# Twenty more unread matmuls in TensorE's program of a fused attention and mixture-of-experts kernel

## The chip, the cores and the metric

The kernel runs on one core of one Trainium2 chip. The metric is the device time of one execution in microseconds (us); lower is better. Five engines work side by side, each on its own instruction list, and meet through semaphores: TensorE (PE, with its weight loads shown as PEld), VectorE (DVE), ScalarE (ACT), GpSimd (POOL) and SyncE (SP, which issues most transfers here).

The chip grants TensorE's clock at one of two levels, 2.4 GHz or half of it, 1.2 GHz. The profile shows it as PEclk: 1.00 is 2.4 GHz, 0.50 is 1.2 GHz.

## The reference

Three stages feed each other: banded attention, a top-1 mixture of eight experts with a skip score, and a dense mixture of four experts.

```python
# attention: q, k, v are (2, 8, 768, 64)
scores = scale * np.matmul(q, k.transpose(0, 1, 3, 2))
scores = scores + bias[None, :, :, :]          # -slope * distance
scores = np.where(keep, scores, -1000000000.0)  # 8 global keys, 96 local ones
a = softmax(scores); attn_out = np.matmul(a, v)
x = attn_out.transpose(0, 2, 1, 3).reshape(B * S, H * D)   # 1536 x 512
# first mixture: rows with x @ w_skip > 0
e_idx = np.argmax(xc @ w_gate, axis=1)
y[mask] = gate_w[mask, None] * (np.maximum(xc[mask] @ w1[e], 0.0) @ w2[e])
out[do_compute] = xc + y
# second mixture: every row through all four experts
for e in range(E):
    out += p[:, e:e + 1] * (np.maximum(x @ w1[e], 0.0) @ w2[e])
```

## The kernel before

**Attention** works through 48 units `u`: eight groups `n` (two heads of one batch element) of six query tiles `i` each. For each unit TensorE does `scores` (L1841; each product three times, for the high and low parts of keys and queries), `probs_T` (transposes of the softmaxed tile, L1850) and `pv` (probabilities times values, L1865 and L1866). Between them stand `fill` (transposes of the next keys and queries, L1815), `outputs_T` (transposes of three finished output tiles, L1874) and `logits` (the gate's nine columns, L1884). VectorE masks and normalises; ScalarE takes exponentials and copies.

**The end of attention** is a chain that no other unit covers. VectorE's `normalise` (L1261 to L1268) makes the last three output tiles, TensorE transposes them (`outputs_T(NB - 1, 1)`), ScalarE copies the transposes to SBUF (L923), TensorE multiplies them with the gate weights (`logits(NB - 1, 1)`) and VectorE adds the result to the rest (L1289).

**The routing** follows. VectorE takes the argmax of the logits (L1422 to L1428). TensorE counts each token's rank in its expert (L1952 and L1955, thirteen small matmuls). VectorE makes twelve one-hot tiles of the ranks (L1438), TensorE turns them into lists of tokens (L1962, 24 matmuls of 8 columns) while they come, and GpSimd gathers the tokens of each expert from DRAM (L825). In the meantime TensorE collects the gate weights (L1971). The gathered rows are transposed (L2001), copied by ScalarE (L1010) and go through the experts.

**The first mixture** runs as blocks of twelve 512-column matmuls (L2032) on weight pieces that VectorE and ScalarE split into a high and a low part (L1174, L902). A piece's buffer is loaded again by SyncE once TensorE's block is done (L646). **The second mixture** is L2133 and L2154; it fills the time from about 250 us to the end, almost all on TensorE.

Each engine runs its list in the order in which the code is written; a waiting instruction holds back everything behind it on its engine. There is no planner.

`unread(n)` (L1793 to L1797) issues `n` matmuls of 512 columns in bf16, with `ones_b` as both operands. They write PSUM bank 3, and what they write is read by nobody. The kernel before calls it with 9 at the very start, with 3 and 7 behind the scores of units 0 and 1. Eight more of the same kind, written out at L1968 (five) and L1975 (three), write bank 7. Bank 3 also takes the transposed probabilities of odd units and later the rank counts.

`banded(pe)` waits until VectorE has computed a flag (L1201) and then reads it into a register; the branch `pe.If(f > 0)` follows it.

Of the kernel before, what the change touches and what calls it, by code (L numbers as in the profile page):

```python
# [25 lines left out]
P = 128  # L26
# [6 lines left out]
def build(nc, q, k, v, n_global, n_local, w_skip, w_gate, m1_w1, m1_w2, probs, m2_w1, m2_w2, out, t_d, xz_d):  # L33
# [4 lines left out]
    DM = H * D  # L38
    KD = DM // P
    E, _, F = m1_w1.shape  # L40
    KF = F // P
    E2 = m2_w1.shape[0]
# [18 lines left out]
    with ctx:  # L61
# [3 lines left out]
        def sb(name, shape, dt):  # L65
            return ctx.enter_context(nc.sbuf_tensor(name, shape, dt))
# [6 lines left out]
        ones_b = sb("ones_b", [P, P], BF16)  # L73
# [280 lines left out]
        ps = ctx.enter_context(nc.psum_tensor("ps", [P, 8, 512], F32))  # L354
# [175 lines left out]
        def banded(eng):  # L530

            eng.wait_ge(bias_ready, 1)
            return eng.value_load(flags[0:1, 0:1], min_val=0, max_val=1)

        def wait(eng, s, value):

            if not isinstance(value, int) or value > 0:
                eng.wait_ge(s, value)
# [39 lines left out]
        def group_bank(n, g):  # L578
            j = place[n, g]
            return 4 + j if j < 4 else 6 + j % 2  # L580
# [16 lines left out]
        def pt_count(u):  # L597

            return sum(by_act(w) == by_act(u) for w in range(u + 1))

        def pt_sem(u):
            return pt_act if by_act(u) else pt_dve
# [1187 lines left out]

        @block.tensor
        def _(pe):
            def unread(n):  # L1793

                for x in range(n):
                    pe.matmul(ps[:, 3, :].rearrange("p (a c) -> p a c", c=P), ones_b[:, :],  # L1796
                              ones_b[:, :].unsqueeze(1).broadcast_to([P, 4, P]), start=True, stop=True)  # L1797

            pe.wait_ge(const_p, 1)
            unread(9)  # L1800
            pe.wait_ge(const_p, 4)

            def bank_free(j):
                if j >= 4:
                    group_out(pe, j - 2)

            def transposed(n, g, src, loaded):
                c, bank = int(g[1]), group_bank(n, g)
                bank_free(place[n, g])
                if (n, c) == (0, 0):  # L1810
                    pe.wait_ge(ld_first["kq".index(g[0])], 32)
                else:
                    pe.wait_ge(loaded[n % 2], (n // 2) * 32 + 32)
                for x, t in enumerate(tiles(n, c)):
                    mm = pe.transpose(ps[:, bank, x * P:(x + 1) * P], src[n % 2][:, t, :], ident[:, :])  # L1815
                mm.then_inc(tr_done, 1)

            def fill(n, g):
                if g[0] == "k":
                    transposed(n, g, kn, ld_k)  # L1820
                else:
                    transposed(n, g, qn, ld_q)
# [30 lines left out]
            def pv(u):  # L1853
                n, i = u // NI, u % NI
                b, half = n % 2, i // 3
                if i == 0:
                    pe.wait_ge(ld_v[b], (n // 2) * 96 + 96)
                if i % 3 == 0 and n:
                    pe.wait_ge(o_done, 2 * n - 1 + half)
                pe.wait_ge(pt_sem(u), pt_count(u))  # L1860
                for h in range(2):
                    out_ = ps[:, 4 + half, (i % 3 * 2 + h) * VW:(i % 3 * 2 + h + 1) * VW]
                    if i:
                        prev = vn[b][:, 0, h, :] if i == 1 else vp[b][:, i - 2, h, :]
                        pe.matmul(out_, pt_sb[u % 3][:, 2 * h, :], prev, start=True, stop=False)  # L1865
                    mm = pe.matmul(out_, pt_sb[u % 3][:, 2 * h + 1, :], vn[b][:, i, h, :], start=(i == 0), stop=True)  # L1866
                mm.then_inc(pv_done, 1)

            def outputs_T(n, half):
                g = "xb" if half else "xa"  # L1870
                bank_free(place[n, g])
                pe.wait_ge(o_done, 2 * n + 1 + half)
                for x in range(3):
                    mm = pe.transpose(ps[:, group_bank(n, g), x * P:(x + 1) * P], xo[n % 2][:, 3 * half + x, :], ident[:, :])  # L1874
                mm.then_inc(tr_done, 1)

            def logits(n, half):
                pe.wait_ge(xo_cp, 2 * n + 1 + half)
                if not half and not n:
                    pe.wait_ge(ld_small, 48)  # L1880
                if not half:
                    wait(pe, lg_add, n)
                for t in range(3 * half, 3 * half + 3):
                    mm = pe.matmul(ps[:, 4, LG + t * (E + 1):LG + (t + 1) * (E + 1)], xoT[:, t, :], wg9[:, n // 2, :], start=True, stop=True)  # L1884
                mm.then_inc(lg_mm, 1)

            fill(0, "k0")
            fill(0, "q0")
            f = banded(pe)
            with pe.If(f > 0):  # L1890
                fill(0, "k1")
                fill(0, "q1")
                pe.wait_ge(v_ones, 4)
                for u in range(NU_):
                    n, i = u // NI, u % NI
                    scores(u)
                    if filled(u):
                        fill(*filled(u))
                    if u >= 1:
                        probs_T(u - 1)  # L1900
                    if n and i in (0, 3):
                        outputs_T(n - 1, i // 3)
                    if n and i in (1, 4):
                        logits(n - 1, i // 3)
                    if u >= 2:
                        pv(u - 2)
                    if u < 2:
                        unread((3, 7)[u])
                outputs_T(NB - 1, 0)
                probs_T(NU_ - 1)  # L1910
                pv(NU_ - 2)
                logits(NB - 1, 0)
                pv(NU_ - 1)
                outputs_T(NB - 1, 1)
                logits(NB - 1, 1)
            with pe.Else():
                pe.wait_ge(ld_small, 48)
                with pe.Fori(0, NI * B * H) as n:
                    pe.wait_ge(g_ld, n * 48 + 48)
                    pe.transpose(ps[:, 0, P:2 * P], ident[:, :], ident[:, :])  # L1920
                    pe.transpose(ps[0:D, 0, 0:P], g_q, ident[:, :])
                    for c in range(NI):
                        mm = pe.transpose(ps[0:D, 1 + c // 4, (c % 4) * P:(c % 4 + 1) * P], g_k[:, c, :], ident[:, :])
                    mm.then_inc(g_t, 1)
                    pe.wait_ge(g_c, n + 1)
                    pe.matmul(ps[:, 3, :], g_qT[0:D, :], g_kT[0:D, 0:512], start=True, stop=True)
                    pe.matmul(ps[:, 4, 0:S - 512], g_qT[0:D, :], g_kT[0:D, 512:S], start=True, stop=True).then_inc(g_sd, 1)
                    pe.wait_ge(g_ex, n + 1)
                    for c in range(NI):
                        mm = pe.transpose(ps[:, 5 + c // 4, (c % 4) * P:(c % 4 + 1) * P], g_p[:, c * P:(c + 1) * P], ident[:, :])  # L1930
                    mm.then_inc(g_pt, 1)
                    pe.wait_ge(g_pc, n + 1)
                    for c in range(NI):
                        mm = pe.matmul(ps[:, 7, 0:D], g_pT[:, c, :], g_v[:, c, :], start=(c == 0), stop=(c == NI - 1))
                    mm.then_inc(g_pv, 1)


                pe.wait_ge(gx_ready, 1)
                for t in range(NT + 1):
                    if t < NT:  # L1940
                        for c in range(KD):
                            mm = pe.transpose(ps[:, t % 2, c * P:(c + 1) * P], X[:, t, c * P:(c + 1) * P], ident[:, :])
                        mm.then_inc(rt_tr, 1)
                    if t >= 1:
                        pe.wait_ge(rt_cp, t)
                        for c in range(KD):
                            mm = pe.matmul(ps[:, 2, (t - 1) * (E + 1):t * (E + 1)], xT[(t - 1) % 2][:, c, :], wg9[:, c, :],
                                           start=(c == 0), stop=(c == KD - 1))
                mm.then_inc(lg_done, 1)
# [3 lines left out]
            for t in range(NT):  # L1953
                n = NT - t
                mm = pe.matmul(ps[:, 3, (t + 1) * E:(NT + 1) * E].rearrange("p (t e) -> p t e", e=E), ones_b[:, :],  # L1955
                               oh_b[:, t, :].unsqueeze(1).broadcast_to([P, n, E]), start=False, stop=(t == NT - 1))
            mm.then_inc(rk_done, 1)

            for t in range(NT):
                pe.wait_ge(one_done, t + 1)  # L1960
# [237 lines left out]
```

## Time and profile before

| | us |
|---|---|
| median of three runs | 760.8 |
| lowest and highest | 760.09, 762.6 |
| the profiled execution, its own time | 762.36 |
| its span, first to last instruction | 760.6 |
| TensorE busy | 738.0 (97%) |
| VectorE busy | 465.7 (61%) |
| ScalarE busy | 324.7 (43%) |
| mean granted clock of TensorE | 0.983 |

Times in the rows count from the start of the span. A row of the timeline gives start, duration, engine, line, operation, what it writes and reads, how often, and in brackets how long the engine was idle before it and what ended that. Matmul durations include the way through the array, so a few in a row take less than the sum of their single times; the start of the next group shows the pace. A row of the chain gives start, duration and what the end of the span goes back to at that time.

### The profile page before, as it was taken

Reading aid. Unit: us, or ns where it says so; the run is one execution under the profiler, and the core shown is the slowest. Engines: PE = TensorE matmul, PEld = TensorE weight load, DVE = VectorE, ACT = ScalarE, POOL = GpSimd, SP = SyncE. Lnnn points to the kernel's source line nnn. Section 1 sums busy time; section 2 is a strip of 40 time slices with the busy share of each in tenths; the row PEclk is TensorE's granted clock in tenths of the full one; section 3 lists DMA queues with packets and bytes.
Section 4 is the critical chain, followed back from the end, with each engine's and each line's share of the span. In section 5 each row is a group of like instructions: output and inputs, shape, how many; then the busy total and the mean of one; then the engine's idle time right before and its main releaser. Section 6 shows DMA issues by size and latency. Waiting matters only on the chain.

```text
span 760.6 us, 11208 instructions
## 1 busy us (share of the span) xinstructions
PE 738.0 (97%) x4155; PEld 651.0 (86%) x4156; DVE 465.7 (61%) x932; ACT 324.7 (43%) x585; POOL 77.1 (10%) x114
## 2 busy tenths in 40 slices
PE   8999998799999799999999999999999999999996
PEld 4898897577888789899898998988989989899895
DVE  5776765699998966752752654563375275265442
ACT  3665665488987643331340431432333134042130
POOL 3101000116427000000000000000000000000203
PEclk8999999699999999999999999999999999999999
DMA  9769951799967220110020030020011003000102
GB/s 155 169 154 279 254 172 35 248 389 383 341 234 119 43 84 0 56 56 1 1 111 1 1 111 1 1 78 32 0 55 55 0 0 110 0 0 0 56 28 83
DMA packets 85969, 74.11 MB, mean 97 GB/s; under 512 B 52642, under 2 KB 58788, under 8 KB 85924
## 3 DMA queue, kind: packets, MB, share of 16 engines
q1 hardware_dynamic: 81924, 64.97, 28.2%
q0 software_dynamic: 3456, 8.43, 4.4%
q8 instruction: 25, 0.41, 0.2%
q10 hardware_dynamic: 544, 0.13, 0.1%
q14 instruction: 20, 0.16, 0.1%
HBM read 67.19 MB, written 6.33 MB: 97 GB/s over the span
## 4 chain that ended last, share of the span: by engine, by line
PE 89%; DVE 6%; ACT 1%; DMA 1%; issue 1%; SPq 0%; POOLq 0%; POOL 0%; DVEq 0%
PE ps L2154 34%; PE ps L2133 30%; PE ps L2032 9%; PE ps L1841 3%; PE ps L1866 2%; PE ps L1865 2%; PE ps L1850 2%; DVE piece_lo L1174 2%; PE ps L1815 2%; PE ps L1884 1%; PE ps L1874 1%; PE ps L2007 1%; DVE X L1268 1%; DVE ql L1225 1%; PE ps L1796 1%
## 5 line engine op out<-in xcount | busy, mean ns | idle before, releaser
L2133 PE MATMUL ps<-xs,w1s 128*128 128x384 f32 x1344 | 238.9, 337 | 3.8 <-ACT shared L1088 2.7
L2133 PEld LDWEIGHTS ps<-xs,w1s 128*128 128x128 f32 x1344 | 235.0, 189 | 6.6 <-ACT shared L1088 3.2
L2154 PE MATMUL ps<-w2s,h_hi 128*128 128x512 f32 x768 | 237.2, 390 | 0.0
L2154 PEld LDWEIGHTS ps<-w2s,h_hi 128*128 128x128 f32 x768 | 143.8, 188 | 29.1
L2154 PE MATMUL ps<-w2s,h_lo 128*128 128x512 f32 x384 | 149.9, 390 | 0.0
L1723 DVE SCALAR_TENSOR_TENSOR X<-ps,prn,X 128x512 f32<-128x512 f32 x84 | 63.1, 751 | 121.7 <-PE ps L2154 121.3
L1088 ACT ACTIVATE shared<-ps 128x384 f32<-128x384 f32 x96 | 45.8, 488 | 185.0 <-PE ps L2133 185.0
L1692 DVE TENSOR_TENSOR shared<-ps,shared 128x384 f32<-128x384 f32 x96 | 52.3, 556 | 92.7 <-ACT shared L1088 69.5
L2154 PEld LDWEIGHTS ps<-w2s,h_lo 128*128 128x128 f32 x384 | 72.1, 188 | 15.0
L1091 ACT ACTIVATE h_hi<-shared 128x384 fp32r<-128x384 f32 x96 | 49.7, 525 | 36.0 <-DVE shared L1692 36.0
L890 POOL DMA_INDIRECT out<-X,dst_i x12 | 11.6, 966 | 495.1 <-DVE X L1723 495.1
L1174 DVE TENSOR_TENSOR piece_lo<-ring,piece_hi 128x1024 fp32r<-128x1024 f32 x48 | 56.4, 1219 | 2.9 <-ACT piece_hi L902 2.8
L1698 DVE SCALAR_TENSOR_TENSOR h_lo<-shared,h_hi 128x384 fp32r<-128x384 f32 x96 | 50.2, 551 | 2.4 <-ACT h_hi L1091 0.5
L1245 DVE CUSTOM_DVE_ANT_0 area<-ps,shared 128x256 f32<-128x256 f32 (+1 forms) x96 | 34.7, 399 | 27.6 <-PE ps L1841 26.5
L931 ACT ACTIVATE area<-area,shared 128x256 f32<-128x256 f32 (+1 forms) x96 | 41.6, 482 | 21.9 <-DVE shared L1245 21.9
L902 ACT ACTIVATE piece_hi<-ring 128x1024 fp32r<-128x1024 f32 x48 | 48.0, 1057 | 0.0
L997 ACT ACTIVATE w2s<-raw 128x1024 fp32r<-128x1024 f32 x16 | 16.1, 1052 | 70.4 <-PE ps L2154 70.4
L2032 PE MATMUL ps<-piece_hi,xT_r 128*128 128x512 f32 x128 | 35.8, 403 | 1.0 <-ACT xT_r L1010 0.8
L2032 PE MATMUL ps<-piece_hi,hT_r 128*128 128x512 f32 x128 | 35.3, 399 | 1.1 <-DVE hT_r L1523 1.0
L1866 PE MATMUL ps<-X,raw 128*128 128x65 f32 x192 | 35.4, 273 | 0.0
L1865 PE MATMUL ps<-X,raw 128*128 128x65 f32 x160 | 30.1, 270 | 0.0
L2032 PEld LDWEIGHTS ps<-piece_hi,hT_r 128*128 128x128 f32 x128 | 23.3, 188 | 6.9 <-DVE hT_r L1523 2.4
(192 smaller groups left out, 834.0 us busy)
## 6 DMA issues: line engine op xcount, KB each, us to landing
ring<-in_moe_w SPq DMA_DIRECT2D x24, 1024.0 KB, 10.0
raw<-in_moe_w SPq DMA_DIRECT2D x16, 1024.0 KB, 5.1
shared<-in_moe_w SPq DMA_DIRECT2D x8, 1024.0 KB, 9.6
X<-in_v SPq DMA_DIRECT2D x16, 192.0 KB, 2.9
ys_d<-X SPq DMA_DIRECT2D x8, 384.0 KB, 3.3
X<-in_k SPq DMA_DIRECT2D x14, 192.0 KB, 4.1
shared<-in_q SPq DMA_DIRECT2D x14, 192.0 KB, 4.2
X<-in_v SPq DMA_DIRECT2D x16, 96.0 KB, 2.9
```

Of the source, the lines that this page charges most:

```text
L902: act.activation(unit(piece_hi[b % NHI], x), unit(piece_raw[b % NR], x), ACT.Copy).then_inc(p_hi, 1)
L1088: act.activation(part[:, slot, f, :], ps[:, 3 * f + BANK[ITEMS[item][0]], 0:HT], ACT.Copy).then_inc(copied, 1)
L1091: act.activation(h_hi[:, c, second * HT:second * HT + HT], src, ACT.Relu).then_inc(hd_hi, 1)
L1174: dve.tensor_tensor(unit(piece_lo[b % NR], x), unit(piece_raw[b % NR], x), unit(piece_hi[b % NHI], x).bitcast(F32), ALU.subtract).then_inc ...
L1692: dve.tensor_tensor(part[:, slot, f, :], ps[:, 3 * f + BANK[ITEMS[item][0]], 0:HT], part[:, slot, f, :], ALU.add).then_inc(added, 1)
L1698: dve.scalar_tensor_tensor(h_lo[c][:, here], src, 0.0, h_hi[:, c, here].bitcast(F32), ALU.max, ALU.subtract).then_inc(hd_lo, 1)
L1723: dve.scalar_tensor_tensor(X[:, t, :], ps[:, 6 + k % 2, :], p_, X[:, t, :], ALU.mult, ALU.add).then_inc(acc_done, 1)
L1865: pe.matmul(out_, pt_sb[u % 3][:, 2 * h, :], prev, start=True, stop=False)
L1866: mm = pe.matmul(out_, pt_sb[u % 3][:, 2 * h + 1, :], vn[b][:, i, h, :], start=(i == 0), stop=True)
L2032: mm = pe.matmul(ps[:, bank, :], src[xp][:, c0 + c, :], w[wp][:, c, :], start=(x == 0 and c == 0 and not (kind == "B" and half)), stop=(x ...
L2133: mm = pe.matmul(out_, w1s[:, wp, WI[name], c, f * P:(f + 1) * P], xs[:, 3 * b:3 * b + 3, xp, XI[name], c, :], start=(not onto and x == 0 ...
L2154: mm = pe.matmul(ps[:, 6 + k % 2, :], h_, w2s[:, wp, c, :], start=(x == 0 and c == 0), stop=(x == 2 and c == 3))
```

## The change

`unread` gets a second parameter, the PSUM bank, with 3 as its default. The first call issues ten instead of nine. Five calls are new: 2 between the first query transposes and the read of the flag, 3 ahead of the last `outputs_T`, 2 between it and the last `logits`, 9 behind these logits, and 3, on bank 7, behind the rank counts. That is 1 + 2 + 3 + 2 + 9 + 3 = 20 more matmuls. Nothing else moves.

```diff
         @block.tensor
         def _(pe):
-            def unread(n):
+            def unread(n, bank=3):
 
                 for x in range(n):
-                    pe.matmul(ps[:, 3, :].rearrange("p (a c) -> p a c", c=P), ones_b[:, :],
+                    pe.matmul(ps[:, bank, :].rearrange("p (a c) -> p a c", c=P), ones_b[:, :],
                               ones_b[:, :].unsqueeze(1).broadcast_to([P, 4, P]), start=True, stop=True)
 
             pe.wait_ge(const_p, 1)
-            unread(9)
+            unread(10)
             pe.wait_ge(const_p, 4)
...
             fill(0, "k0")
             fill(0, "q0")
+            unread(2)
             f = banded(pe)
             with pe.If(f > 0):
                 fill(0, "k1")
...
                 logits(NB - 1, 0)
                 pv(NU_ - 1)
+                unread(3)
                 outputs_T(NB - 1, 1)
+                unread(2)
                 logits(NB - 1, 1)
+                unread(9)
             with pe.Else():
...
             mm.then_inc(rk_done, 1)
+            unread(3, 7)
 
             for t in range(NT):
                 pe.wait_ge(one_done, t + 1)
```

TensorE's list at the start of the program, before and then after. `X` holds the first keys, `shared` the first queries; `TENSOR_LOAD flags` is the read of the flag.

```order
L1796 MATMUL ps<-ones_b 128x512 x9
L1815 MATMUL ps<-ident,X 128x128 x2
L1815 MATMUL ps<-ident,shared 128x128 x2
L533 TENSOR_LOAD flags
L533 ISA x2
L1890 COMPARE_AND_BRANCH
```

```order
L1796 MATMUL ps<-ones_b 128x512 x10
L1815 MATMUL ps<-ident,X 128x128 x2
L1815 MATMUL ps<-ident,shared 128x128 x2
L1796 MATMUL ps<-ones_b 128x512 x2
L533 TENSOR_LOAD flags
L533 ISA x2
```

One unread matmul more stands ahead of the first key transposes, and two stand between the first query transposes and the flag.

TensorE's list at the end of attention, before and then after. The rows of 65 columns are the last `pv`; L1874 is `outputs_T` and L1884 `logits`, three instructions each (the trace shows the three of `logits` as six). What follows the branch in the list is the other side of the `If`; on this input the engine goes on at the rank counts.

```order
L1865 MATMUL ps<-X,raw 128x65
L1866 MATMUL ps<-X,raw 128x65
L1874 MATMUL ps<-ident,X 128x128 x3
L1884 MATMUL ps<-wg,area 128x9 x3
L1890 UNCONDITIONAL_BRANCH
```

```order
L1865 MATMUL ps<-X,raw 128x65
L1866 MATMUL ps<-X,raw 128x65
L1796 MATMUL ps<-ones_b 128x512 x3
L1874 MATMUL ps<-ident,X 128x128 x3
L1796 MATMUL ps<-ones_b 128x512 x2
L1884 MATMUL ps<-wg,area 128x9 x3
L1796 MATMUL ps<-ones_b 128x512 x9
L1891 UNCONDITIONAL_BRANCH
```

Fourteen unread matmuls now stand around the last transposes and the last logits, nine of them ahead of the branch.

TensorE's list from the last rank counts to the gate weights, before and then after.

```order
L1955 MATMUL ps<-X,ones_b 128x16
L1955 MATMUL ps<-X,ones_b 128x8
L1962 MATMUL ps<-X 128x8 x24
L1968 MATMUL ps<-X,ones_b 128x512 x5
L1971 MATMUL ps<-X 128x24 x12
```

```order
L1959 MATMUL ps<-X,ones_b 128x16
L1959 MATMUL ps<-X,ones_b 128x8
L1796 MATMUL ps<-ones_b 128x512 x3
L1967 MATMUL ps<-X 128x8 x24
L1973 MATMUL ps<-X,ones_b 128x512 x5
L1976 MATMUL ps<-X 128x24 x12
```

Three unread matmuls now stand between the rank counts and the token lists; the five at L1968 stay where they were.

## Rows read from the trace of the kernel before

**Rows 1.** Stages: busy time of each engine (instructions), PEclk, DMA share, GB/s

```profile
0.00:20.00 20.00, 17.02 (x87) 9.82 (x89) 11.41 (x46) 7.88 (x17) 8.11 (x44) 0.83 0.93 147
...
130.00:147.00 17.00, 10.19 (x75) 6.35 (x76) 9.00 (x44) 7.05 (x9) 3.31 (x3) 0.60 0.58 184
...
265.00:760.60 495.60, 489.67 (x2471) 443.06 (x2469) 259.19 (x409) 148.60 (x272) 11.59 (x12) 1.00 0.10 36
```

**Rows 2.** Timeline of TensorE around the last outputs, the logits and the routing

```profile
126.91 0.52 PE L1874 MATMUL ps<-ident,X 128*128 128x128 f32 x3 [0.43 <-DVE X L1268]
...
131.44 0.87 PE L1874 MATMUL ps<-ident,X 128*128 128x128 f32 x3 [1.17 <-DVE X L1268]
132.89 1.45 PE L1884 MATMUL ps<-wg,area 128*128 128x9 f32 x6 [0.58 <-ACT area L923]
137.08 0.27 PE L1952 MATMUL ps<-X,upper_b 128*128 128x104 bf16 x1 [2.74 <-DVE X L1428]
...
138.82 2.00 PE L1962 MATMUL ps<-X 128*128 128x8 bf16 x24 [0.93 <-DVE X L1438]
141.06 1.91 PE L1968 MATMUL ps<-X,ones_b 128*128 128x512 bf16 x4 [0.24 <-issue]
```

**Rows 3.** The chain that ended last, from the last outputs to the first expert

```profile
122.99 0.57 PE ps L1884 x6
...
131.44 0.89 PE ps L1874 x3
...
132.89 1.46 PE ps L1884 x6
...
137.35 0.55 PE ps L1955 x12
...
138.82 2.02 PE ps L1962 x24
...
141.39 3.54 DMA area<-ys_d,tok_i
...
189.33 2.77 PE ps L2032 x12
```

**Rows 4.** Single microseconds, columns as in rows 1: where the granted clock changes

```profile
8.00:9.00 1.00, 0.88 (x5) 0.72 (x4) 0.87 (x3) 0.60 (x1) 0.38 (x2) 0.55 1.22 195
...
14.00:15.00 1.00, 1.00 (x4) 0.35 (x3) 0.88 (x2) 0.00 (x0) 0.80 (x2) 0.54 1.30 204
...
131.00:132.00 1.00, 0.56 (x3) 0.50 (x3) 0.29 (x1) 0.00 (x0) 0.00 (x0) 0.50 0.00 0
...
144.00:145.00 1.00, 0.94 (x4) 0.17 (x2) 0.00 (x1) 0.00 (x0) 0.06 (x1) 0.68 0.56 152
```

**Rows 5.** Timeline of TensorE in the first 16 us

```profile
1.07 3.88 PE L1796 MATMUL ps<-ones_b 128*128 128x512 bf16 x9 [1.07 <-POOL ones_b L756]
5.85 0.41 PE L1815 MATMUL ps<-ident,X 128*128 128x128 f32 x2 [0.90 <-DMA X<-in_k]
...
7.36 0.65 PE L1815 MATMUL ps<-ident,X 128*128 128x128 f32 x4 [0.89 <-DMA X<-in_k]
8.13 1.12 PE L1815 MATMUL ps<-ident,shared 128*128 128x128 f32 x4
...
12.83 2.72 PE L1796 MATMUL ps<-ones_b 128*128 128x512 bf16 x7
15.47 0.39 PE L1841 MATMUL ps<-kh,qh 64*128 64x256 f32 x2
```

**Rows 6.** Timeline of VectorE: two places at the start, and the one-hot tiles

```profile
10.25 0.29 DVE L1245 CUSTOM_DVE_ANT_0 area<-ps,shared 128x128 f32<-128x128 f32 x1 [0.79 <-PE ps L1841]
...
13.87 0.68 DVE L1225 SCALAR_TENSOR_TENSOR ql<-ps,qh 128x512 fp32r<-128x512 f32 x1
...
138.51 2.04 DVE L1438 TENSOR_SCALAR X<-iota_rb,area 128x128 bf16<-128x128 bf16 x12
```

**Rows 7.** Waits of SyncE's queue from 146 to 247 us

```profile
SPq L646 <- PE ps L2032: 48.1, 18, 3.3
```

## The prediction

> **What bounds the kernel now.** I read the stages first: from 265 us to the end TensorE is busy for 489.67 of 495.60 us at a granted clock of 1.00, and the change touches nothing there. Two stretches have a lower clock: the first 20 us (0.83) and 130 to 147 us (0.60), where TensorE is also idle for 6.8 of 17 us [rows 1]. The single microseconds show where the level changes: down at 8.1 us, up at 14.9, down at the start of 131, up in 144 [rows 4]. So 6.9 and 13.7 us run at 1.2 GHz. The chain of waits says what that costs: in 130 to 147 us it alternates between engines, and TensorE's pieces of it (transposes, logits, rank counts, token lists) have no cover [rows 3]. The timeline then gives the pauses into which the new matmuls go [rows 2, 5].
>
> The stages are coupled. An earlier expert stage starts its own transfers earlier, because SyncE loads a piece when TensorE has finished the block that held its buffer; SyncE's queue waits 48.1 us in all for that [rows 7]. Behind it TensorE is full. So I pass a gain ahead of 147 us on to the end at its full size, and a loss as well.
>
> **The price of one unread matmul.** At the low clock nine took 3.88 us, 0.431 each; 512 columns in that time are the 1.2 GHz level, although PEclk has no record of a change there yet [rows 5]. At the high clock no row shows an unread stream alone. The nearest is the expert blocks, twelve matmuls of 512 columns with their weight loads in 2.77 us, 0.231 each [rows 3]; I take it as the price.
> The Trainium skill (TensorE: Matmul & The Clock Gate, section "Wait — 56ns, not 53.3ns?") gives 426.7 ns and 215.7 ns start to start for 512 columns at the two levels. The first agrees with the 0.431 of rows 5; by the second the nine matmuls of the argmax would take an estimated 1.94 us instead of 2.08, and no step below would change sign.
>
> **The start: ten for nine, and two behind the first queries.** The tenth costs 0.23 to 0.43 us and lies in a pause of 0.90 us that ends with the landing of keys. The two cost 0.46 to 0.86 us and lie in the next pause, 0.89 us [rows 5]. Both are covered, by 0.03 us at worst. If the flag's read had to wait for the two, the four key transposes (0.65 us) could come late by some 0.3 us; the query transposes at 8.13 us wait for their own landing, so little of this reaches anyone. I take 0, bounds 0 and +0.3.
> Do they keep the clock from falling at 8.1? Between 5 and 8 us TensorE would still have pauses: of 1.79 us of idle time 0.7 to 1.3 are filled. I think the fall stays in most executions, and take 0 for it here as well; the other case is rival C.
>
> **The last outputs and logits.** In the trace the clock falls at 131.0, inside the 1.17 us for which TensorE waits for the last outputs, so everything behind it is at half speed [rows 2, 4].
> - The transposes take 0.87 us in the timeline; the same three, 0.52 at the high clock [rows 2]. Gain 0.35.
> - The logits take 1.46 us of the chain; the same six, 0.57 at the high clock [rows 3]. Gain 0.89.
> - Three unread ahead of the transposes: 0.69 us in a pause of 1.17, covered; at the low clock 1.29, so +0.12.
> - Two between them: 0.46 us in a pause of 0.58 (ScalarE's copy), covered with 0.12 to spare; at the low clock 0.86, so +0.28. ScalarE needs only the transposes' semaphore and isn't held up.
>
> **The nine during the argmax.** Ready for TensorE 2.74 us behind the logits are the one-hots that VectorE makes of them; that whole path is VectorE's, including a branch, and doesn't change its length. Nine take 2.08 us at the high clock: covered, with 0.66 us for TensorE's own branch behind them. At the low clock they take 3.88 us and the rank counts come 1.14 us late.
>
> **Rank counts and the three behind them.** The counts' chain pieces are 0.27 and 0.55 us [rows 2, 3]. No row has them at the high clock; their time falls between nothing and half, so 0 to 0.4, and I take 0.25, since both ratios above (0.52 to 0.87, 0.57 to 1.46) are large. Three unread behind them: 0.69 us in a pause of 0.93 in which VectorE turns ranks into one-hots; at the low clock 1.29, so +0.36. The 24 token-list matmuls take 2.02 us beside VectorE's twelve one-hots of 2.04 us [rows 3, 6]: VectorE sets that pace. 0 to 0.2, I take 0.1. The gather of 3.54 us behind them is a transfer [rows 3]: 0.
>
> **Sum.** If the clock is held from the last outputs through the rank counts: 0.35 + 0.89 + 0.25 + 0.10 = 1.59 us, with all 20 matmuls under cover. Against the profiled execution, 762.36 us, that is 760.8. The profiled execution is near the slowest of those known (760.09 to 762.6) and 1.56 above the median. Its clock fell almost as early as it could, 0.9 us behind the last attention matmul; an execution in which it falls later has less to win back. I give the median two thirds of the sum, 1.1 us: 760.8 - 1.1 = 759.7.
>
> **Rivals.**
> A, the forecast: held through the logits in most executions. 759.7, own range 759.0 to 760.5. For it: the longest pause of the stretch shrinks from 1.17 to 0.5 us, the pause of the argmax from 2.74 to 0.7.
> B, no measurable effect: 760.8, within 0.4. The clock may fall all the same between 130 and 137 us in about as many executions as before, since the transposes still wait for VectorE and ScalarE. Or it is held but falls at some 138 us, behind the rank counts, and is still low when the first expert starts: the row at 144 us shows it rising only just ahead of that [rows 4]. A low stretch of 3.4 us, half of the first one's 6.9, at 0.431 for 0.231 would cost 3.4 x 0.46 = 1.6 us, and take the gain back.
> The Trainium skill (same page, section "What's actually happening") describes the gate as free-running and not reset by a kernel's start, so that the moment of a change varies between runs. By that rule one trace can't promise the same 131.0 us for the next execution; the times of before, 2.5 us apart, agree with it, and it is why I cut the sum.
> C, the start is held too. Then the query transposes take 0.65 instead of 1.12 us and VectorE, idle for 0.79 us until the first scores, begins up to 0.75 us earlier; it is then busy until 14.55 (13.87 + 0.68) with what the third scores need, which begin at 15.47 only because seven unread at the low clock stand ahead of them (2.72 us; 1.6 at the high one). They could begin at 13.85: a gain of 1.6 us [rows 5, 6]. Time: 759.7 - 1.6 = 758.1. Against it: the pauses between 5 and 8 us are not filled.
> D, the other side: the clock is lost at 131 us as now and the nine are issued at 0.431. They leave cover at 2.74 / 9 = 0.304 us each, between both prices. Then the ranks are late by 1.14 us, and with the smaller overruns (0.12 + 0.28 + 0.36) by 1.90, and the routing, the gather and every expert with them. As the stream of nine may itself bring the clock back I take 1.5: 762.3.
>
> **How the numbers follow.** A 0.48, B 0.26, C 0.13, D 0.13. The likeliest is A: 759.7 us. About 0.3% (2.3 us) is what a measurement of this kernel can tell from no change: below 758.5 is faster, above 763.1 slower. C gives nearly all of faster, with the best executions of A: 0.18. D reaches 763.1 only in its worst form: 0.06. The rest, 0.76, is the same. The range from 758.0 to 762.3 takes in C's and D's values and leaves out their far ends.
>
> **What would show it.** PEclk at 1.00 from 131 to 137 us; the last transposes at about 0.5 us, the logits at 0.6; the pause ahead of the rank counts gone down to some 0.7 us, ended by VectorE still; the first expert 1.6 us earlier against the end of attention. If the rank counts follow the nine unread without a pause, D holds. If the clock is 0.50 at the first expert block, B's second form does. If the third scores begin near 14 us, C does. I am wrong altogether if the expert stage, started earlier, waits for weights: then TensorE would show idle time ended by transfers between 147 and 247 us, which it doesn't have now.

## The result and the profile after

The changed kernel takes 762.98 us (median of 20 executions, 759.47 to 764.28), the kernel before 761.53 in the same number (759.81 to 762.68). The ratio is 1.0018, with a 95% interval of 1.0009 to 1.0026: slower by 0.1 to 0.3%, outside the range that was predicted, where a gain of 1.1 us had been forecast. The profiled execution took 762.91 us, its span is 761.2.

The first 15 us went better than forecast. Timeline of TensorE of the changed kernel, same columns as [rows 5]:

```profile
5.80 0.61 PE L1815 MATMUL ps<-ident,X 128*128 128x128 f32 x2 [0.28 <-DMA X<-in_k]
...
6.47 0.59 PE L1796 MATMUL ps<-ones_b 128*128 128x512 bf16 x2
7.37 0.65 PE L1815 MATMUL ps<-ident,X 128*128 128x128 f32 x4 [0.31 <-issue]
8.10 0.66 PE L1815 MATMUL ps<-ident,shared 128*128 128x128 f32 x4
...
14.10 0.39 PE L1841 MATMUL ps<-kh,qh 64*128 64x256 f32 x2 [1.19 <-DVE ql L1225]
```

The keys' transposes start within 0.05 us of [rows 5]; the query transposes take 0.66 us instead of 1.12, and the third unit's scores start at 14.10 instead of 15.47, now 1.19 us after TensorE was ready for them. The clock isn't lost at 8 us.

The end of attention and the routing, answering to [rows 2]:

```profile
128.72 0.81 PE L1796 MATMUL ps<-ones_b 128*128 128x512 bf16 x3
130.05 0.52 PE L1874 MATMUL ps<-ident,X 128*128 128x128 f32 x3 [0.52 <-DVE X L1268]
130.40 0.59 PE L1796 MATMUL ps<-ones_b 128*128 128x512 bf16 x2
131.15 0.84 PE L1884 MATMUL ps<-wg,area 128*128 128x9 f32 x6
131.84 2.10 PE L1796 MATMUL ps<-ones_b 128*128 128x512 bf16 x9
134.73 0.22 PE L1956 MATMUL ps<-X,upper_b 128*128 128x104 bf16 x1 [0.79 <-DVE X L1428]
...
136.21 2.00 PE L1967 MATMUL ps<-X 128*128 128x8 bf16 x24 [0.26 <-DVE X L1438]
138.28 1.02 PE L1973 MATMUL ps<-X,ones_b 128*128 128x512 bf16 x4
140.67 0.49 PE L1976 MATMUL ps<-X 128*128 128x24 bf16 x12 [1.37 <-DVE X L1453]
141.01 1.44 PE L1980 MATMUL ps<-X,ones_b 128*128 128x512 bf16 x3
142.63 1.12 PE L2006 MATMUL ps<-ident,area 128*128 128x128 f32 x4 [0.18 <-DMA area<-ys_d,tok_i]
144.52 2.04 PE L2037 MATMUL ps<-piece_hi,xT_r 128*128 128x512 f32 x4 [0.78 <-ACT xT_r L1010]
146.37 1.91 PE L2037 MATMUL ps<-piece_lo,xT_r 128*128 128x512 f32 x4
```

All new matmuls are under cover: pauses of 0.52, 0.79 and 0.26 us are left, each ended by VectorE. But the first two groups of four 512-column matmuls of the first expert take 2.04 and 1.91 us, where before has 1.16 and 1.08. The stages tell why (columns as in [rows 1]):

```profile
130.00:144.00 14.00, 10.88 (x83) 5.57 (x84) 7.40 (x39) 6.67 (x9) 2.37 (x2) 0.83 0.71 221
144.00:148.00 4.00, 3.48 (x8) 2.81 (x9) 3.59 (x4) 0.38 (x1) 0.94 (x1) 0.50 0.92 312
148.00:152.00 4.00, 4.00 (x18) 3.20 (x17) 1.64 (x2) 0.87 (x2) 0.00 (x0) 0.80 1.01 386
```

The clock is at 2.4 GHz through the argmax and the rank counts, falls at 139.4 us, in the pause of 1.37 us ahead of the gate weights, and is at 1.2 GHz until 149.6 us, through the first five microseconds of the experts. The chain of waits gives each step its size. Of the changed kernel:

```profile
130.05 0.53 PE ps L1874 x3
...
131.15 0.85 PE ps L1884 x6
...
134.95 0.35 PE ps L1959 x12
...
136.21 2.01 PE ps L1967 x24
...
138.78 3.81 DMA area<-ys_d,tok_i
...
142.63 1.13 PE ps L2006 x4
...
144.52 6.73 PE ps L2037 x18
```

And of the kernel before, the two pieces of its chain that [rows 3] doesn't have:

```profile
144.98 0.68 PE ps L2001 x4
...
146.42 4.35 PE ps L2032 x18
```

| step | before | after | difference, us |
|---|---|---|---|
| last attention matmul ends (VectorE starts on it) | 130.29 | 128.89 | -1.40 |
| last transposes | 0.89 | 0.53 | -0.36 |
| last logits | 1.46 | 0.85 | -0.61 |
| rank counts | 0.82 | 0.57 | -0.25 |
| token lists | 2.02 | 2.01 | -0.01 |
| first gather, issue to landing | 3.54 | 3.81 | +0.27 |
| transposes of the gathered rows | 0.68 | 1.13 | +0.45 |
| 18 matmuls of the first expert | 4.35 | 6.73 | +2.38 |
| sum | | | +0.47 |

The transposes that follow start at 151.25 instead of 150.77: +0.48, so the table is complete to 0.01 us. 2.6 us are won ahead of the gather, and 3.1 given back in it and behind it.

The table compares two executions, and their spans differ by 0.6 us only (760.6 and 761.2), while the medians differ by 1.45. The profiled execution of before is one of its longer ones (its median span is 759.6), that of the changed kernel is close to its median (761.25). So some 0.9 us of the measured loss lies in the shorter executions of before, and of those there is no trace.

The 20 executions point the same way. Each one's span stands with its mean granted clock:

| kernel | mean clock: executions, spans in us |
|---|---|
| before (35 executions) | 0.990: 14, 758.1 to 759.1; 0.986: 13, 759.3 to 760.1; 0.988: 1, 761.2; 0.983: 7, 760.3 to 760.8 |
| changed (20 executions) | 0.997: 1, 757.7; 0.993: 5, 760.4 to 760.6; 0.991: 3, 759.5 to 761.5; 0.990: 3, 761.1 to 761.5; 0.988 and less: 8, 761.2 to 762.5 |

At 0.990, about 15 us recorded at the low level in both, the changed kernel's spans are 2.0 to 3.4 us longer. That points to what TensorE has to do while the clock is low, and not to how long it is low. The one execution in which it hardly fell is the fastest.

The mean clock needs care: the record has no entry before its first change and shows 1.00 until then. In the trace of the kernel with only the 17 matmuls from the last outputs on (below), TensorE's timeline has

```profile
7.36 1.11 PE L1815 MATMUL ps<-ident,X 128*128 128x128 f32 x4 [0.41 <-DMA X<-in_k]
...
14.97 0.38 PE L1841 MATMUL ps<-kh,qh 64*128 64x256 f32 x2
```

so these key transposes run at half speed (0.65 us in [rows 5]), and the seven unread matmuls at 12.9 us still take 2.14 us, where the changed kernel has 1.67 and before 2.72. The clock is low until about 14 us, an estimate from these three, and the record has no low entry there. The trace of before with 11 more shows the same. Low microseconds at the start can be missing from the mean clock of other executions too.

### The profile page after: what moved, and what is told of

It reads as the page before. It is cut to its first block, busy times and chain, and to the rows that moved or that the text cites. A ratio compares the mean times of both kernels' runs of the same rounds, so it can differ in the third digit from the quotient of the medians.

```text
span 761.2 us, 11248 instructions
## 1 busy us (share of the span) xinstructions
PE 741.0 (97%) x4175; PEld 651.9 (86%) x4176; DVE 465.7 (61%) x932; ACT 324.7 (43%) x585; POOL 77.2 (10%) x114
## 4 chain that ended last, share of the span: by engine, by line
PE 89%; DVE 7%; ACT 1%; DMA 1%; issue 1%; POOLq 0%; DVEq 0%; POOL 0%; SPq 0%
PE ps L2159 34%; PE ps L2138 30%; PE ps L2037 9%; PE ps L1841 3%; PE ps L1866 2%; PE ps L1865 2%; DVE piece_lo L1174 2%; PE ps L1850 2%; PE ps L1815 1%; PE ps L1884 1%; PE ps L1874 1%; PE ps L2012 1%; DVE ql L1225 1%; DVE X L1268 1%; DMA area<-ys_d,tok_i 1%
## 5 line engine op out<-in xcount | busy, mean ns | idle before, releaser
L2159 PEld LDWEIGHTS ps<-w2s,h_hi 128*128 128x128 f32 x768 | 143.7, 188 | 29.2
L2037 PE MATMUL ps<-piece_hi,xT_r 128*128 128x512 f32 x128 | 37.5, 418 | 1.0 <-ACT xT_r L1010 0.8
L2037 PEld LDWEIGHTS ps<-piece_hi,xT_r 128*128 128x128 f32 x128 | 24.0, 198 | 6.4 <-issue 1.1
```

What stands on the lines that cost most here:

```text
L2037: mm = pe.matmul(ps[:, bank, :], src[xp][:, c0 + c, :], w[wp][:, c, :], start=(x == 0 and c == 0 and not (kind == "B" and half)), stop=(x ...
L2159: mm = pe.matmul(ps[:, 6 + k % 2, :], h_, w2s[:, wp, c, :], start=(x == 0 and c == 0), stop=(x == 2 and c == 3))
```

## The experiments

Three theories were set against each other. Theory 1: the change holds the clock where little work is, and moves the low stretch onto the first experts, where work is dense. Theory 2: the added matmuls hold somebody up. Theory 3: an earlier expert stage waits for its weights. Spans are medians over the executions of one job; before has 759.6 in the first two, 759.4 and 758.9 in the later ones.

**The parts alone.** Only the start's three:

```diff
-            unread(9)
+            unread(10)
...
             fill(0, "q0")
+            unread(2)
```

> Only the ten for nine and the two behind the first queries; everything behind the last attention matmul is as before. Theory 1 (the clock is low when the first expert blocks start, because it was kept up earlier and then fell): the start gives back 1.2 to 1.6 us where it holds the clock, the pattern of the routing is that of the kernel before, so the clock rises again ahead of the experts; faster than before by 0.5 to 1.5 us, ratio 0.998 to 0.9993. Theory 2 (the added matmuls at the start hold up the flag's read or the first keys): same or slower, up to +0.5 us. Theory 3 (an earlier expert stage waits for its weights): no gain, ratio 1.000, with idle time of TensorE ended by transfers behind 145 us.

Measured: 762.94 us, ratio 1.0020 (1.0005 to 1.0036), median span 761.2. That is 1.4 us slower than before, which none of the three theories had expected. The profiled execution was one of the best, span 758.0: the start held, the clock fell at 131.6 us and was back at 141.9, and the experts began at full speed. TensorE's timeline:

```profile
143.06 0.66 PE L2002 MATMUL ps<-ident,area 128*128 128x128 f32 x4 [0.59 <-DMA area<-ys_d,tok_i]
144.50 1.17 PE L2033 MATMUL ps<-piece_hi,xT_r 128*128 128x512 f32 x4 [0.78 <-ACT xT_r L1010]
145.50 1.08 PE L2033 MATMUL ps<-piece_lo,xT_r 128*128 128x512 f32 x4
```

But five of the twelve had spans of 762.3 to 762.8 at a clock of 0.982. One trace couldn't say why, so the same kernel was traced twice more.

> A second look at the kernel with the start's three matmuls alone, whose trace had a span of 758.0 us while 5 of its 12 executions had 762.3 to 762.8 at a mean clock of 0.982. If the loss is a low clock at the first experts, an execution of the slow kind shows the routing's low stretch reaching beyond 145 us, some 20 us long, with the start held at 1.00. If it is the start itself (a second low stretch there), the last attention matmul comes at 130 us or later.

> The same as the look before it, once more, since the place of the clock's changes differs from execution to execution: one of the two should be of the slow kind, with the routing's low stretch reaching into the experts (first theory) or a low stretch in the first 20 us (second).

The first of the two had the start held, a fall at 130.0, a rise at 143.7, transposes of the gathered rows at 143.58 and a span of 759.2. The second was one of the long ones, span 762.6, clock 0.982. Its timeline:

```profile
138.92 2.29 PE L1969 MATMUL ps<-X,ones_b 128*128 128x512 bf16 x5
141.52 0.50 PE L1972 MATMUL ps<-X 128*128 128x24 bf16 x12 [0.31 <-DVE X L1453]
141.86 1.44 PE L1976 MATMUL ps<-X,ones_b 128*128 128x512 bf16 x3
143.63 1.11 PE L2002 MATMUL ps<-ident,area 128*128 128x128 f32 x4 [0.33 <-DMA area<-ys_d,tok_i]
145.52 2.05 PE L2033 MATMUL ps<-piece_hi,xT_r 128*128 128x512 f32 x4 [0.78 <-ACT xT_r L1010]
```

and its stages:

```profile
144.00:148.00 4.00, 3.22 (x10) 2.37 (x9) 2.59 (x3) 0.60 (x1) 0.94 (x1) 0.50 0.80 244
148.00:152.00 4.00, 4.00 (x11) 3.13 (x11) 2.64 (x3) 0.60 (x1) 0.00 (x0) 0.57 1.04 390
```

This is the telling pair with the trace of before: in both the clock falls at 131.0 us. In before it is back at 144.6 us, during the last of the eight unread matmuls of L1968 and L1975, which run from about 141 to 144.9 us with one pause of 0.31 [rows 2, 4]. Here the same eight come 1.7 to 2.1 us earlier, from 138.9 to 143.3, two pauses (0.33 and 0.78 us) follow, and the clock is back at 151.5 only. The 18 matmuls of the first expert take 7.10 us of the chain instead of 4.35. So the start's gain is real, and the loss of this execution is theory 1's. But in the other two traces of this kernel the same eight, just as early, had the clock back in time (141.9 and 143.7 us). Five of the twelve executions have spans like this one's, 762.3 us and more, and of the 35 of before none is above 761.2; so with the three at the start the eight seem to fail more often. Only this one of the long ones was traced, and why they fail more often when they come earlier is not shown.

Only the 17 from the last outputs to the rank counts:

```diff
                 pv(NU_ - 1)
+                unread(3)
                 outputs_T(NB - 1, 1)
+                unread(2)
                 logits(NB - 1, 1)
+                unread(9)
...
             mm.then_inc(rk_done, 1)
+            unread(3, 7)
```

> Only the 17 matmuls from the last attention outputs to the rank counts; the start is as before. Theory 1: the logits and rank counts gain 1.0 to 1.6 us, then the clock falls at the token lists or the gather and the first expert blocks run at 1.2 GHz, costing 1.5 to 3 us; slower than before by 1 to 2 us, ratio 1.001 to 1.003, and the low stretch of the clock lies over the first expert blocks in the trace. Theory 2: the nine overrun their pause at the low clock and the rank counts come up to 1.1 us late, with no pause ahead of them. Theory 3: a gain of 1.2 us up to the gather that is lost between 145 and 175 us with the clock at 1.00.

Measured: 764.05 us, ratio 1.0034 (1.0022 to 1.0045), median span 762.3: by its ratio the worst of the parts, and somewhat worse than theory 1 had expected. In its trace the clock was low from 140.1 to 150.4 us and the gathered transposes took 1.11 us, the first four expert matmuls 2.05. The rank counts had a pause of 0.78 us ahead of them, so the nine overrun nothing, and theory 2 falls here.

Only the three and the two around the last transposes:

```diff
                 pv(NU_ - 1)
+                unread(3)
                 outputs_T(NB - 1, 1)
+                unread(2)
                 logits(NB - 1, 1)
```

> Of the change only the three and the two around the last transposes; no matmuls at the start, none of the nine and none behind the rank counts. If it is the keeping up of the clock into the rank counts that puts the next low stretch over the experts, this has a fall some 3 to 7 us earlier than with the nine and mostly rises before the experts: as fast as before or up to 1 us faster, median 760.5 to 761.5. If any earlier routing meets the low clock at the experts (the clock's changes are not tied to the program), this is slower than before too, by 0.5 to 2 us.

Measured: 764.10 us, ratio 1.0027 (1.0011 to 1.0044), median span 762.25. The milder form of theory 1 was wrong: it doesn't need the nine. The loss, 2.9 us against before in the same job, is larger than either form of the expectation allowed. In its trace the clock fell at 133.9 us and was low until 150.9:

```profile
138.84 2.29 PE L1970 MATMUL ps<-X,ones_b 128*128 128x512 bf16 x5
141.44 0.49 PE L1973 MATMUL ps<-X 128*128 128x24 bf16 x12 [0.31 <-DVE X L1453]
141.78 1.44 PE L1977 MATMUL ps<-X,ones_b 128*128 128x512 bf16 x3
143.67 1.12 PE L2003 MATMUL ps<-ident,area 128*128 128x128 f32 x4 [0.45 <-DMA area<-ys_d,tok_i]
```

**The price of a low clock at the experts.** The kernel before without its eight unread matmuls:

```diff
-            for x in range(5):
-                pe.matmul(ps[:, 7, :], ones_b[:, :], onehot[:, 0:4, :], start=True, stop=True)
...
-            for x in range(3):
-                pe.matmul(ps[:, 7, :], ones_b[:, :], onehot[:, 0:4, :], start=True, stop=True)
```

> The kernel before without its eight unread matmuls between the token lists and the gathered rows, so that nothing brings the clock up ahead of the experts; all real work is the same and at the same times up to the gather. Theory 1: the clock is 0.50 for the first 3 to 5 us of the expert blocks, which puts a price on it alone: slower than before by 1.5 to 3 us, ratio 1.002 to 1.004. Theories 2 and 3: within 0.5 us of before.

Measured: 763.56 us, ratio 1.0028 (1.0017 to 1.0039), median span 761.8. Up to the gather its timeline is that of before to 0.01 us; the clock was low from 131.1 to 151.6 us. Its chain:

```profile
144.98 1.13 PE ps L2001 x4
...
146.87 6.54 PE ps L2032 x18
```

1.13 + 6.54 against 0.68 + 4.35 is 2.64 us, with nothing added anywhere. That is the price of theory 1 by itself, and nearly the 2.83 us (0.45 + 2.38) of the changed kernel.

**Keeping the clock into the experts.** The changed kernel with 11 more:

```diff
-            for x in range(5):
+            for x in range(10):
...
-            for x in range(3):
+            for x in range(6):
...
             x_transposed(0)
+            unread(3, 7)
```

> The changed kernel with 11 unread matmuls more behind the token lists: ten for five while VectorE makes the gate's parts, six for three ahead of the gather's landing, three between the first transposes of the gathered rows and the first expert block. Theory 1: the clock stays at 1.00 into the experts and the whole gain is kept, 757.5 to 759 us beside 761.5 of before, ratio 0.995 to 0.998. Theory 2: as slow as the changed kernel or slower, since more is queued. Theory 3: the clock is held and the time still does not move below 760.5.

Measured: 760.43 us, ratio 0.9987 (0.9976 to 0.9999), median span 758.7: 2.5 us shorter than the changed kernel's 761.25, by adding work. It is less than the 757.5 to 759 us that theory 1 had expected: against before in the same job the median gains 1.1 us. Theory 3 falls too: the experts begin at 144.50 us at full speed and TensorE has no idle time ended by a weight transfer behind them. The same with 8 more (eight for five, five for three, three):

> The changed kernel with 8 more instead of 11: eight for five, five for three, three behind the gathered transposes. In the trace with ten for five these ran at the low clock and held up the gate-weight matmuls and the gathered transposes by some 0.5 us. If that overrun matters, this is 0.3 to 0.6 us faster than the version with 11 (span median 758.7), 758.2 us in span. If the clock is lost at the experts more often with fewer, its slower executions reach spans of 761 us and the median rises.

Measured: 760.49 us, ratio 0.9989 (0.9980 to 0.9998), median span 758.7. No gain from fewer. In both traces the clock still fell at the token lists (137.3 and 137.0 us), and the unread ones behind them ran at 0.43 us each while it was low, until 140.7 and 143.8 us. Timeline of the version with 8:

```profile
138.06 3.57 PE L1973 MATMUL ps<-X,ones_b 128*128 128x512 bf16 x8
141.42 0.52 PE L1976 MATMUL ps<-X 128*128 128x24 bf16 x12
```

The gate-weight matmuls start at 141.42 us without a pause; in the changed kernel they started at 140.67 after 1.37. That overrun is theory 2's mechanism, real here at 0.75 us; the gathered transposes start at 143.84, some 0.8 us behind the landing of the gather.

The kernel before with the same 11 and none of the 20:

> The kernel before with only the 11 unread matmuls that the changed kernel got in the experiment before (ten for five, six for three, three between the gathered transposes and the first expert block), none of the 20 of the change. If the low clock at the first experts is the only thing that the 11 mend, before, which mostly reaches the experts at the high clock by itself, gains little: 760.5 to 761.5 us, ratio 0.999 to 1.0, and the 20 are worth the 1 to 2 us between this and the held changed kernel. If the 11 bring the whole gain, this is as fast as that one, 759 to 760.4 us.

Measured: 761.73 us, ratio 1.0006 (0.9996 to 1.0016), median span 759.95. The 11 alone bring nothing. One reason is the expected one, that before mostly reaches the experts at the high clock; its trace shows a second one. There the clock was low from 133.2 to 143.4 us, and the ten for five took 4.43 us:

```profile
143.32 0.50 PE L1971 MATMUL ps<-X 128*128 128x24 bf16 x12
...
144.96 0.60 PE L2001 MATMUL ps<-ident,area 128*128 128x128 f32 x4
```

The gate-weight matmuls start 4.1 us behind the end of the token lists (139.24) without a pause, where before needs 2.5, and the gathered transposes start some 1.0 us behind the landing of the gather (issued at 139.8, 4.1 us in flight). The experts met the high clock and started no earlier than in before (146.34 and 146.42 us). So the 11 need the 20 to gain anything, and part of the reason is that in this trace they met the low clock and overran.

**All pauses filled up to the experts:**

```diff
             for t in range(NT):
                 pe.wait_ge(one_done, t + 1)
+                if t % 2:
+                    unread(1, 7)
...
-            for x in range(5):
+            for x in range(9):
...
-            for x in range(3):
+            for x in range(5):
...
             x_transposed(0)
+            unread(3, 7)
```

> The changed kernel with unread matmuls in all pauses up to the experts: one behind every second one-hot (six, between the token lists), nine for five behind the lists, five for three ahead of the gathered rows, three behind their transposes. In the traces with 8 and 11 more the clock still fell during the token lists (137.0, 137.3 us) and the ones behind them, at 0.43 each, held up the gate weights by 0.7 us. Theory 1: with the lists' pauses filled it stays at 1.00 from 8 us to 260 us, span median 757.5 to 758.3, ratio 0.995 to 0.998, the best of all. Against it: the six slow the lists, which VectorE paces at 0.17 us a tile, by up to 0.5 us and nothing is won over the versions with 8 and 11 (758.7).

Measured: 760.50 us, ratio 0.9986 (0.9976 to 0.9995), median span 758.75. The clock was held from about 6 us to 258.3 us, but the median is that of the two versions before it and misses the 757.5 to 758.3 that theory 1 had expected. Where the rest of the gain stays, the chain says:

```profile
138.99 4.15 DMA area<-ys_d,tok_i
```

The gather is issued 2.40 us earlier than in before and lands 1.79 us earlier. Where the chain goes through it, its flight was 3.54 us (issued at 141.4, in two traces), 3.61 (140.2), 3.75 (139.3), 3.81 (138.8), 3.96 (139.6), 4.08 (139.5), 4.15 and 3.62 (both 139.0) and 4.49 (139.6). Every earlier one took longer, by up to 0.95 us, but the moment of the issue alone doesn't set it: the two of 139.0 us are 0.53 us apart with the same program up to there. What it meets is not shown.

The profiled execution is also the longest of the twelve (span 760.2, the others 758.2 to 759.0), and its timeline shows a second loss:

```profile
258.97 11.43 PE L2141 MATMUL ps<-xs,w1s 128*128 128x384 f32 x48 [2.67 <-ACT shared L1088]
```

The clock is low from 258.3 to 265.1 us, over the first dense matmuls of the second mixture. The kernel of the last experiment below has the same 48 at the high clock: they start at 258.42 us and end at 267.91, 9.49 us with a pause of 0.59 in them, 1.9 us less.

The same without the start's three:

> The same as the run before it but without the ten-for-nine and the two at the start. With the experts safe in both, the difference is the start's own worth: theory 1 expects 1.0 to 1.5 us slower than with them (the scores of the third unit at 15.5 instead of 14.1 us in most executions), though alone they made the kernel slower. If the start's matmuls are bad in themselves, this is the faster one.

Measured: 761.40 us, ratio 1.0004 (0.9993 to 1.0014), median span 759.65, so 0.9 us longer than with them. The three that made the kernel slower alone are worth 0.9 us once the experts are safe.

**The next pause of the same kind**, at the start of the second mixture, where the clock fell at 258 to 264 us in eleven of the thirteen other traces:

```diff
                     elif name == "P4":
+                        if begin and not b and not f:
+                            pe.wait_ge(s_made, 3)
+                            unread(10, 7)
                         pe.wait_ge(copied, by_step(m, half, b, 6, 3 + f))
```

> The changed kernel with all pauses filled up to the experts (as the run before the last) and ten unread matmuls more in the 2.7 us for which TensorE waits for ScalarE at the start of the second mixture (258 us), in which the clock falls in most traces. If a fall there costs what it does in the routing, this gains 0.7 to 1.3 us over the version without the ten (span median 758.75): span median 757.5 to 758.1, and the low stretch at 258 to 265 us is gone. If the ten start late (they wait for VectorE's last read of the bank they write) or meet the low clock, they overrun the pause by up to 1.6 us: span median 759 to 760.5.

Measured: 759.87 us, ratio 0.9985 (0.9974 to 0.9995), median span 758.1, against 758.75 without the ten. Its timeline and its stages:

```profile
255.58 2.33 PE L1796 MATMUL ps<-ones_b 128*128 128x512 bf16 x10
258.42 6.54 PE L2144 MATMUL ps<-xs,w1s 128*128 128x384 f32 x36 [0.50 <-ACT shared L1088]
```

```profile
130.00:147.00 17.00, 14.87 (x111) 8.49 (x113) 10.46 (x43) 7.05 (x9) 3.31 (x3) 1.00 0.71 234
247.00:261.00 14.00, 12.35 (x67) 9.94 (x66) 12.49 (x29) 10.04 (x24) 0.59 (x1) 1.00 0.14 20
261.00:265.00 4.00, 3.96 (x23) 3.63 (x21) 4.00 (x8) 1.39 (x3) 0.00 (x0) 1.00 0.72 231
```

The clock is 1.00 in all of them. All twelve executions have spans between 757.7 and 758.4 us, where before has 758.1 to 761.3 in the same job. The median is 0.8 us below that of before there (760.68 us) and 3.1 below that of the changed kernel in its own job (762.98). The version does so by cutting off the long executions; the best ones of before are within 0.4 us of its best.

## Why the prediction was wrong

**The step that failed: the sum has no term for the clock at the first expert.** It ends at the token lists and takes everything behind them at the speed that it has in before. The runs showed +0.45 us for the gathered transposes and +2.38 for the first 18 expert matmuls, 2.83 us in place of nothing. The mechanism was there as rival B's second form, weighed too low: a clock held past the argmax that falls at some 138 us and is still low at the first expert. The trace after has exactly that, with the fall at 139.4. It was given a share of 0.26 with the harmless form of B, and priced at 1.6 us on a stretch of 3.4 us. The stretch in the experts was 5.1 us of 10.2, and its price 2.83 us; 2.64 by the experiment that has nothing else in it. [rows 4] had shown the clock rising at 144 us, less than two microseconds ahead of the experts. I read that as a cost of before that ends in time. It should have been read as a condition on which before rested, met in its trace by eight matmuls at L1968 and L1975 whose place in time the change moves.

**The starting point.** The forecast counted from 760.8 us, the median of three executions; with 20 the median of before is 761.53. So 0.7 us of the miss lies there; the change that was forecast, -1.1 us, measured +1.45.

**The start.** I took 0 because the pauses between 5 and 8 us were not all filled. They were filled enough: the clock held in the trace after and in all the seven others of kernels with the three matmuls, and in none of the six without them. Rival C's sum of 1.6 us measured 1.37 at the third scores and 1.40 at the end of attention: they wait for VectorE until 14.10 us and not, as C had it, until about 13.85. The mechanism was right, the chance of 0.13 was not.

**Outputs, logits, rank counts.** 0.35 for the transposes measured 0.36. 0.89 for the logits measured 0.61, so this term was mis-sized: the six take 0.85 us of the chain at the high clock when they follow a short pause. The 0.57 of [rows 3] is from a place where they follow other matmuls without one; the chain counts there only what lies behind the matmul before, and the timeline has 0.73 us for them. 0.25 for the rank counts measured 0.25. 0.10 for the token lists measured 0.01; VectorE sets their pace.

**The nine** needed no more than their pause: 0.79 us were left where 0.66 was forecast (the path through VectorE kept its 2.74 us, and the nine, 2.10 us long, start 0.15 us ahead of the end that the profile gives the logits). Rival D didn't happen in any trace of a kernel with the nine.

**The gather** was put down at 0 because it is a transfer. It gave back 0.27 us here and up to 0.95 elsewhere; the cause is open.

**Passing the gain on at full size** was right, and so was passing on a loss: +0.48 us at 151 us is +0.6 at the end of the span. No weights were waited for.

**The cut to two thirds**, for a fall that comes at another moment in another execution, asked the right question of the wrong place. The variation mattered most for whether the clock is back at the experts. (The fall in before comes 0.7 us behind the end of the last attention matmul, 130.29 us, and not 0.9.) Three traces of one and the same kernel (the start's three alone) have falls at 131.6, 130.0 and 131.0 us, rises at 141.9, 143.7 and 151.5, and spans of 758.0, 759.2 and 762.6 us. The Trainium skill (TensorE: Matmul & The Clock Gate, section "What's actually happening") calls the gate free-running, not reset when a kernel starts, so that the point of a transition varies; the three traces agree.

## What to carry to other kernels

A low stretch of TensorE's clock costs what TensorE has to do in it: 13.7 us over a routing with few small matmuls cost 1.2 us, about 5 us over dense blocks 2.8. Before matmuls are added to hold the clock up in thin work, look at what follows it, and fill every pause up to the dense work or leave the thin work slow and bring the clock back right ahead of the dense one. Matmuls that bring the clock back in one execution can fail in the next one: of three traces of one kernel the same eight did it in two. One trace of such a kernel shows one draw, so set the spans of many executions beside their mean clock, and remember that this mean can miss a low stretch at the start.

## What the runs showed of the hardware

A nine-matmul stream of 512 columns in bf16 takes 2.10 us at 2.4 GHz, and a single one 0.38 to 0.39, so about 0.21 us from start to start; at 1.2 GHz it is 0.43 (eight in 3.57 us, three in 1.44). The Trainium skill (TensorE: Matmul & The Clock Gate, section "Wait — 56ns, not 53.3ns?") states 215.7 and 426.7 ns, and the traces agree.

In all eight traces of kernels with the three unread matmuls at the start TensorE is at the high clock from about 6 us on, and the third scores start between 14.07 and 14.12 us. In the six traces without them it is at the low clock from about 8 us to 11 us or later, and those scores start between 14.63 and 15.52.

With the clock held everywhere the spread of twelve executions fell from some 3 us to 0.7: most of what looked like noise between executions of this kernel goes with the clock's changes. Not all of it is accounted for: one execution of the version without the start's three has a recorded clock of 0.997 and a span of 761.0 us, and there is no trace of it.
